# Hidden rows of the expert layer turned by VectorE in 32x32 squares instead of by TensorE

## The reference

```python
logits = xn @ en.T / tau                      # 1536 tokens, 8 experts
expert_idx = np.argmax(logits, axis=1)
gate_w = probs[np.arange(N), expert_idx]
for e in range(E):
    mask = expert_idx == e
    h = np.maximum(x[mask] @ w1[e], 0.0)      # w1: 512 x 1024
    out[mask] = gate_w[mask, None] * (h @ w2[e])   # w2: 1024 x 512
```

## Time and profile before

| | |
|---|---|
| median of three runs | 525.04 us (524.76 to 525.34) |
| profiled execution | 524.4 us, of which the span (first to last instruction) is 522.7 us |
| TensorE busy | 510.8 us, 98% of the span |
| VectorE, ScalarE, GpSimd busy | 332.8, 212.7, 92.6 us |
| mean granted TensorE clock | 0.998 of full |
| share of TensorE in the chain that ended last | 95% |

### The profile page before, as it was taken

The page is one execution under the profiler, slowest core; times in us unless marked ns, Lnnn a source line. Parts: engine busy times, 40 slices in busy tenths (PEclk is TensorE's granted clock), DMA queues, the critical chain, the costliest instruction groups (busy, mean ns, idle before and its releaser), DMA issues.

```text
span 522.7 us, 11557 instructions
## 1 busy us (share of the span) xinstructions
PE 510.8 (98%) x3754; PEld 440.2 (84%) x3755; DVE 332.8 (64%) x712; ACT 212.7 (41%) x480; POOL 92.6 (18%) x223
## 2 busy tenths in 40 slices
PE   8899999999999999999999999999999999999994
PEld 7688888888888888888898988887788888888883
DVE  3779897788876665666654578677573473222662
ACT  5677753443443334333422545440532441111440
POOL 6413131003240000000000001003221211111221
PEclk9999999999999999999999999999999999999999
DMA  8999425587454336332423610102864145101000
GB/s 213 279 334 285 89 56 101 131 152 135 107 129 86 67 66 146 66 66 43 120 42 133 231 41 22 61 3 93 334 250 144 40 184 192 40 29 37 20 20 25
DMA packets 125899, 60.24 MB, mean 115 GB/s; under 512 B 95382, under 2 KB 113814, under 8 KB 125856
## 3 DMA queue, kind: packets, MB, share of 16 engines
q1 hardware_dynamic: 123456, 53.38, 37.8%
q0 software_dynamic: 2400, 6.30, 3.6%
HBM read 50.22 MB, written 11.01 MB: 117 GB/s over the span
## 4 chain that ended last, share of the span: by engine, by line
PE 95%; ACT 1%; issue 1%; DMA 1%; SPq 0%; DVE 0%; POOLq 0%; DVEq 0%; ACTq 0%
PE bank L1050 26%; PE bank L1094 9%; PE bank L1101 9%; PE bank L1107 9%; PE bank L1257 5%; PE bank L1303 5%; PE bank L1265 5%; PE bank L1311 5%; PE bank L1305 5%; PE bank L1259 5%; PE bank L1028 3%; PE bank L998 2%; PE bank L1295 2%; PE bank L1162 1%; PE bank L1007 1%
## 5 line engine op out<-in xcount | busy, mean ns | idle before, releaser
L1458 ACT ACTIVATE el<-bank 128x512 f32<-128x512 f32 x48 | 28.6, 596 | 90.5 <-PE bank L1050 90.2
L1050 PE MATMUL bank<-x_hi,w_hi_parts 128*128 128x256 f32 x376 | 60.5, 283 | 0.0
L1050 PE MATMUL bank<-x_hi,w_lo_parts 128*128 128x256 f32 x376 | 60.2, 282 | 0.0
L1050 PE MATMUL bank<-x_lo,w_hi_parts 128*128 128x256 f32 x376 | 60.1, 282 | 0.0
L1782 DVE TENSOR_SCALAR el<-el 128x512 f32<-128x512 f32 x48 | 20.4, 425 | 59.9 <-ACT el L1458 59.9
L1050 PEld LDWEIGHTS bank<-x_hi,w_hi_parts 128*128 128x128 f32 x376 | 54.1, 188 | 4.1 <-issue 0.2
L1094 PE MATMUL bank<-w_hi_parts,g_hi 128*128 128x512 f32 x192 | 54.5, 405 | 0.0
L1101 PE MATMUL bank<-w_lo_parts,g_hi 128*128 128x512 f32 x192 | 52.6, 395 | 0.0
L1107 PE MATMUL bank<-w_hi_parts,g_lo 128*128 128x512 f32 x192 | 52.4, 394 | 0.0
L789 POOL COPY kb<-kT 128x96 f32<-128x96 f32 x96 | 26.5, 317 | 142.1 <-PE bank L998 120.6
L1050 PEld LDWEIGHTS bank<-x_lo,w_hi_parts 128*128 128x128 f32 x376 | 51.4, 189 | 0.0
(11 more groups left out here) (292 smaller groups left out, 892.1 us busy)
## 6 DMA issues: line engine op xcount, KB each, us to landing
raw<-in_moe_w SPq DMA_DIRECT2D x8, 2048.0 KB
w_raw<-in_moe_w_in SPq DMA_DIRECT2D x8, 512.0 KB, 6.1
w_raw<-in_moe_w_out SPq DMA_DIRECT2D x8, 512.0 KB, 6.6
p_rows<-p_all SPq DMA_DIRECT2D x16, 256.0 KB, 2.4
p_squares<-p_rows SPq DMA_DIRECT2D x64, 64.0 KB, 2.3
v_raw<-in_v SPq DMA_DIRECT2D x8, 384.0 KB, 4.1
x_rows<-x SPq DMA_DIRECT2D x6, 512.0 KB, 3.2
x<-x_rows SPq DMA_DIRECT2D x20, 128.0 KB, 2.7
```

The source lines that it names most:

```text
L1050: mm = pe.matmul(o, r32(w[:, at:at + P]), r32(x[i % 2][:, c, :]), start=(part == "hh" and c == 0), stop=(part == "lh" and c == DC - 1))
L1458: act.activation(el[n % 2], bank[:, H_BANK[n % 2], :], ACT.Exp).then_inc(e_act, 1)
```

## The change

In slots 2 to 13 TensorE's `transpose_h` is gone. VectorE turns the 128x1024 hidden rows out of PSUM with one instruction that transposes each 32x32 block in its place (`turn_h`, into `h_sb`). To complete the turn, the blocks have to change groups of 32 partitions: 16 moves of 32 partitions x 256 elements (`h_square`), 9 by VectorE (`BY_DVE`) and 7 by ScalarE (`BY_ACT`), each with the ReLU in it, into `h_turned_rows`. ScalarE makes `hT_hi` and VectorE `hT_lo` from there (`h_high`, `h_low`). Slots 0 and 1 keep TensorE's turn.

The hidden columns come out in another order, so the rows of w2 are loaded in that order, in four transfers of 32 partitions in place of one of 128. `transpose_x(3)` now stands inside `up(2)`, and `up(3)` runs half by half (`up_by_halves`). On VectorE `store_y(1)` now stands ahead of `store_xsT(3)`. The table has another row (`STARTS_DOWN`): w1 of a run is split three slots ahead of its start (two before), w2 still one slot ahead.

```diff
+    BY_DVE, BY_ACT = SQUARES[0:9], SQUARES[9:16]
...
+        def h_square(r, q):
+            return (h_turned_rows[q * SQ:(q + 1) * SQ, r * GROUPS_OF_F:(r + 1) * GROUPS_OF_F],
+                    h_sb[r * SQ:(r + 1) * SQ, q * GROUPS_OF_F:(q + 1) * GROUPS_OF_F])
...
-                sp.dma_start(raw[:, W1SZ:WSZ].rearrange("p (c n) -> p c n", c=FC2),
-                             w2[bass.ds(ex, 1)].rearrange("o (c p) n -> p (o c) n", p=P)).then_inc(ld_w2, 16)
+                for r in range(GROUPS):
+                    sp.dma_start(raw[r * SQ:(r + 1) * SQ, W1SZ:WSZ].rearrange("p (c n) -> p c n", c=FC2),
```

On TensorE:

```diff
+            up(FILL)
+            up_by_halves(FILL + 1)
+            transpose_x(FILL + 2)
+            down(FILL)
             with pe.Fori(FILL + 1, NSLOT) as s:
                 with pe.If(s < used):
-                    transpose_h(s)
                     with pe.If(s + 1 < used):
                         transpose_x(s + 2)
                         up(s + 1)
                     down(s)
```

On ScalarE:

```diff
+            def move_h(s):
+                act.wait_ge(h_turned, s)
+                act.wait_ge(hT_ev, 2 * s + 2)
+                for r, q in BY_ACT:
+                    to, of = h_square(r, q)
+                    ins = act.activation(to, of, ACT.Relu)
+                ins.then_inc(moved_a, 1)
...
             with act.Fori(FILL, NSLOT) as s:
                 with act.If(s < used):
-                    hT_high(s)
+                    move_h(s)
+                    h_high(s)
+                    there, run = starting_run(act, s + 1, STARTS_DOWN)
                     with act.If(there > 0):
                         high_w2(run())
+                    there, run = starting_run(act, s + 3)
                     with act.If(there > 0):
+                        act.wait_ge(h1_mm, s + 2)
                         high_w1(run())
-                    with act.If(s + 1 < used):
-                        relu(s + 1)
```

On VectorE:

```diff
+            def turn_h(s):
+                dve.wait_ge(h1_mm, s + 1)
+                dve.wait_ge(moved_a, s - FILL)
+                dve.transpose(h_sb, bank[:, 0:2, :].rearrange("p a n -> p (a n)")).then_inc(h_turned, 1)
...
+            with dve.Fori(FILL, NSLOT) as s:
                 with dve.If(s < used):
+                    h_low(s)
+                    with dve.If(s + 1 < used):
+                        turn_h(s + 1)
+                        move_h(s + 1)
+                        store_xsT(s + 2)
+                    there, run = starting_run(dve, s + 1, STARTS_DOWN)
+                    with dve.If(there > 0):
+                        low_w2(run())
+                    there, run = starting_run(dve, s + 3)
+                    with dve.If(there > 0):
+                        low_w1(run())
                     load_gate(s)
                     dve.wait_ge(g_cp, s + 1)
                     store_y(s, gate_cur[:, 0:1])
```

More of the change, by code:

```diff
@@ L160, in build @@
     SQ = 32
+    GROUPS_OF_F = F2 // GROUPS
+    SQUARES = [(r, q) for r in range(GROUPS) for q in range(GROUPS)]
+    BY_DVE, BY_ACT = SQUARES[0:9], SQUARES[9:16]
     O_TURNS = sorted([(q_at(u), 0, u) for u in STEADY if PAIRS < u < BY_SQUARES]
@@ L325, in build @@
          _, _, emb, emb_n,
-         h_sb, hT_hi, hT_lo, slot_vals, _, xs_even) = zone(
+         h_sb, hT_hi, hT_lo, slot_vals, _, xs_even, _, h_turned_rows) = zone(
             "x",
@@ L1279, in up @@
                 pe.wait_ge(xs_hi_v, s + 1)
-                pe.wait_ge(h1_ev, s + 1)
+                if isinstance(s, int) and s == FILL:
+                    pe.wait_ge(h1_ev, FILL + 1)
+                else:
+                    pe.wait_ge(h_turned, s - 1)
                 for c in range(DC):
@@ L1289, in up, with up_by_halves @@
                     up_low(range(HALVES), base).then_inc(h1_mm, 1)
+            def up_by_halves(s):
+                run, base = run_of(pe, s)
+                pe.wait_ge(xs_hi_v, s + 1)
+                pe.wait_ge(xs_ev, s + 2)
+                pe.wait_ge(h_half_turned, 1)
+                for a in range(HALVES):
+                    if a == 1:
+                        pe.wait_ge(h_turned, FILL)
+                    for c in range(DC):
+                        if a == 0:
+                            pe.wait_ge(raw_lo1, QUARTERS * run + (c + 1))
+                        up_high(c, (a,), base, s)
+                    mm = up_low((a,), base, s)
+                mm.then_inc(h1_mm, 1)
             def transpose_h(s):
@@ L1588, in relu, with relu_half @@
                 act.wait_ge(h1_mm, s + 1)
[L1589 to L1592, removed]
+                act.wait_ge(h1_t, 2 * s)
+                relu_half(0)
+                relu_half(1).then_inc(h1_ev, 1)
+            def relu_half(a):
+                rows = h_sb.rearrange("p (c q f) -> p q c f", c=FC2, q=GROUPS)[:, 2 * a:2 * a + 2, :, :]
+                return act.activation(rows, bank[:, a, :].rearrange("p (q c f) -> p q c f", q=2, c=FC2), ACT.Relu)
             def hT_high(s):
@@ L1599, in hT_high, with h_high @@
                              ).then_inc(hT_hi_a, 1)
+            def move_h(s):
[5 more added lines that the diff above has]
+                ins.then_inc(moved_a, 1)
+            def h_high(s):
+                act.wait_ge(moved_a, s - 1)
+                act.wait_ge(moved_d, s - 1)
+                act.wait_ge(h2_mm, s + 1)
+                for a in range(2):
+                    act.copy(r32(of_half(hT_hi, a)), h_by_chunk(a)).then_inc(hT_hi_a, 1)
             def high_w1(run):
@@ L1921, in store_xsT @@
                 dve.wait_ge(xs_t, s + 1)
-                if not isinstance(s, int) or s > 0:
+                if not isinstance(s, int) or s in (1, FILL):
                     dve.wait_ge(h1_mm, s)
-                hi, lo = (x.rearrange("p c n -> p (c n)") for x in (xsT_hi, xsT_lo))
+                hi, lo = (x.rearrange("p c n -> p (c n)") for x in homes_of_turned_rows(s))
                 dve.tensor_copy(r32(hi), bank[:, bank_of_rows(s), :]).then_inc(xs_hi_v, 1)
@@ L2149, in _ @@
                 low_w2(1)
-            store_xsT(3)
             store_y(1, list_gate[:, 0, 1:2])
+            dve.wait_ge(meta_v, 2)
+            store_xsT(FILL + 1)
+            dve.wait_ge(h1_half, 2)
+            dve.wait_ge(h1_t, 2 * FILL)
+            half = F2 // HALVES
+            dve.transpose(h_sb[:, 0:half], bank[:, H1[0], :]).then_inc(h_half_turned, 1)
+            dve.wait_ge(h1_mm, FILL + 1)
+            dve.transpose(h_sb[:, half:F2], bank[:, H1[1], :]).then_inc(h_turned, 1)
+            dve.wait_ge(h_half_turned, 1)
+            dve.wait_ge(r_mm, NB)
+            move_h(FILL)
             there, run = starting_run(dve, slice(3, 4))
@@ L2154, in _ @@
                 low_w1(run())
[L2155 to L2163 removed]
+            there, run = starting_run(dve, slice(4, 5))
+            with dve.If(there > 0):
+                low_w1(run())
             def load_gate(s):
```

123 lines of the change are left out of this document (67 added, 56 removed).

## The result

The changed kernel takes 542.5 us (median of four runs), the kernel before 525.19 on the same chip: ratio 1.0326, 95% interval 1.0304 to 1.0348. It is slower, as forecast, but by 3.3% where 1.8% was forecast, and outside the range (525 to 541) by 1.5 us.

The account below looks back on a forecast made before the run. TensorE, 98% busy, was taken to bound the kernel. Transposes removed -8.7, loop stalls +11.0, tail +5.5, start +0.6, clock +0.9: +9.3 us on the median 525.04, so 534 us (531 to 539 at 0.55), range 525 to 541.

Parts of the forecast that it names:

- turn of 128x1024: VectorE's `turn_h` in each slot: 1.21 us, with 2.05 as bound.
- nine squares: VectorE's moves of 32x256 behind the turn: 0.30 us each without overlap, 2.65 us for nine.
- VectorE's idle before a w2 split: VectorE between the end of `store_xsT` and the low parts of w2: 1.08 us for table reads.
- gap before `down(13)`: TensorE waits 7.1 us between `down(12)` and `down(13)` for `store_y(12)`, where it was 1.62.
- start (`store_y(1)`): At the start, `store_y(1)` waits for the first scatter ahead of `store_xsT(3)`, so `up(3)` starts later: +0.6 us.
- stalls in the loop: TensorE's waits in iterations 2 to 11, mostly from weight splits delaying `store_y` and the next turn: +11.0 us.
- TensorE's own part of the slot: In loop slots, `transpose_x` through `up` stays at 6.01 us; nothing added.
- clock: After the idling in the tail TensorE comes back slower: +0.9 us, half of 1.8; all of `down(13)` slow would be +5.6.
- rival of 0.20: VectorE's squares overlap, 0.20 us each, chain 0.75 shorter in every slot: +3.3 us in all, 528; chance 0.22.
- the part on the plain slot: Slot without a weight split: VectorE's chain takes 5.5 us, TensorE wants `transpose_x` after 5.58: 0.1 us lost a slot.
- TensorE's busy time down by about 9 us: Sign expected in the profile after, with no matmuls on `h_sb` left in the loop.
- The tail: Iteration 12 splits w2 of weight run 3 with no `up` following to hide it: +5.5 us.

Follow-up runs that it names:

- halves: Changed kernel with each of VectorE's nine squares cut into two of 32x128; one execution for its trace, 547.97 us.
- read_first: Changed kernel with TensorE's table read of `up(s+1)` put ahead of `transpose_x(s+2)`; 538.68 us, ratio 1.0270 to the kernel before.
- xs_first: Changed kernel with VectorE's `store_xsT(s+2)` put ahead of its nine squares; 530.67 us, ratio 1.0119 to the kernel before.
- four: Changed kernel with 4 squares on VectorE and 12 on ScalarE in place of 9 and 7; 529.13 us, ratio 1.0100 to the kernel before.
- tail: Changed kernel with the w2 split of weight run 3 moved from iteration 12 to 11; 536.91 us, ratio 1.0243 to the kernel before.
- b5: b1 with the w2 split of weight run 3 moved from iteration 12 to 11; 518.16 us, ratio 0.9881 to the kernel before.
- b1: Changed kernel with xs_first, read_first and four together, and `store_y(1)` back behind `store_xsT(3)` and the half turns; 521.61 us, ratio 0.9951 to the kernel before.
- y_first: Changed kernel with VectorE's `load_gate` and `store_y` of slot s put ahead of the weight splits; 538.95 us, ratio 1.0278 to the kernel before.
- b2: b1 with the low parts of w2 right behind `h_low(s)`, ahead of the turn; 527.54 us, ratio 1.0078 to the kernel before.
- b3: b1 with the gate and `store_y` ahead of the splits on VectorE; 523.54 us, ratio 0.9982 to the kernel before.

## Why the prediction was wrong

**The direction and most of the mechanism were right**: no gain in TensorE's waiting to be had, a chain on VectorE from the end of `up(s+1)` to `store_y(s)`, stalls in the slots with splits, a tail gap. Its pieces:

| step | predicted | measured |
|---|---|---|
| turn of 128x1024 | 1.21 | 1.25 |
| nine squares | 2.65 | 2.66 |
| VectorE's idle before a w2 split | 1.08 | 1.20 |
| gap before `down(13)` | 7.1 | 7.4 |
| ScalarE's seven squares | 2.6 | 2.97 |
| start (`store_y(1)`) | +0.6 | +0.65 |
| stalls in the loop | +11.0 | +7.9 |
| TensorE's own part of the slot | 0 | +7.7 |
| clock | +0.9 | +3.7 |

**The rule on squares held.** The Trainium skill ("VectorE: DVE Perf Modes", section "Two Vector instructions with no wait between them") says that an instruction in another group of 32 partitions is held until all earlier ones have finished. The squares start 0.296 us apart and last 0.283, and `halves` shows 0.22 with and 0.145 without a change of partitions. The prediction's 0.30 a square stands, and its rival of 0.20 falls. Its reason is not quite right: it says that each square reads and writes other partitions than the last, but up to four in a row read the same ones, and only where they write changes. The trace agrees with the rule as cited, by which either is enough.

**The step that failed** is in the part on the plain slot: "TensorE wants its `transpose_x` 5.58 after the end of `up`, and needs some 0.2 to react: 0.1 us lost a slot." It took the rest of TensorE's slot, 6.01 from `transpose_x` through `up`, as fixed, and priced a late `xsT_lo` at the wait for it alone. But the sequencer's read of `tab` stands behind that wait. With `transpose_x` released only when TensorE gets to it the read can't start sooner, and each slot pays 0.81 more, 7.7 us in the loop. read_first shows that this is the read, xs_first and four that it is paid only while `xsT_lo` comes late: they have no transposes of `h_sb` either and pay nothing. The eight transposes would have given the read 0.87 us more time; the prediction removed them at their full cost and counted no such loss. By the same step its sign "TensorE's busy time down by about 9 us" failed: it fell by 1.

**The stalls of the loop** were over-estimated as a consequence. TensorE was 0.8 us later in each slot, so `y_sb` was less late for it. With the read moved away (read_first) the stalls are 12.6 us against the 11.0 forecast, so the stepping through the slots was near for the TensorE that it assumed. One error thus partly hid the other: together they are 15.6 where 11.0 stood.

**The clock** is the second term that was mis-sized: +0.9 predicted for the tail, +2.2 measured there. Nothing was put down for `up(3)`, where a wait of 2.0 us was followed by another 1.5 lost. The prediction's 3.6 us at half clock were the better figure than the half of it that was taken: in `down(13)` the granted clock is 0.50 for over 4 us. It read them from the distance of matmuls at the start of the program alone; the table of stretches gives a granted clock of 1.00 there (0 to 4 us). By the Trainium skill ("TensorE: Matmul & The Clock Gate", section "HAM oscillation — how this bites in real kernels"), as the prediction told it, the whole 1.8 would have been lost in the tail; the trace shows that and a little more. Not every wait of some us did so: 3.1 us before `up(3)` in `tail` and 2.1 before `down(13)` in b5 cost nothing.

**The tail** was right in mechanism and in size (5.5 and 5.8), and `tail` and b5 show how much of it is the place of one split: the wait falls from 7.25 to 3.27 us, and from 4.64 to 2.10.

What stays open: the +1.1 us up to `up(2)`, which come and go between variants with the same code, and why a wait of two or three microseconds lowers the clock in one place and not in another (below).

## What to carry to other kernels

Before removing work from the bound engine, list what its sequencer does between the instructions, reads of registers from memory first: a read behind an instruction whose wait ends only as the engine gets there is paid (here 0.81 us a slot), so read ahead of the wait, or let what it waits for come earlier. When work goes to a second engine in program order, put there first what the bound engine wants soonest (here the next slot's rows, 2.7 us earlier for a swap of two lines), and move big jobs without a deadline, such as splits of weights, to an iteration that has something to hide them. Such edits win together: none of the single ones beat the kernel before, while b1 and b5 do. Reordering alone can also only move a wait: y_first, b2 and b3 took from one place what they gave in another.

## What the runs showed of the hardware

- A read of a table in SBUF by an engine's sequencer cost TensorE 0.81 us a slot where nothing covered it. On VectorE two in a row cost 1.2 to 1.4 us and three 2.1 (changed), behind the squares 0.4 to 0.7 and 1.35 (xs_first), and two 0.2 to 0.6 in b1.
- A square of 32x256, SBUF to SBUF, takes 0.415 us on ScalarE and 0.283 on VectorE; the turn of 128x1024 out of PSUM takes 1.25 us on VectorE.
- The clock after a wait, by how long `down(13)` then took (5.8 us at full clock) and by `up(3)` to `transpose_x(4)` (5.6):

| wait before it, us | kernel, phase | time of the phase, us |
|---|---|---|
| 0.7 | b1, `up(3)` | 5.6 |
| 2.0 | changed, `up(3)` | 7.2 |
| 2.4 | xs_first, `up(3)` | 7.1 |
| 2.4 | halves, `up(3)` | 5.6 |
| 3.1 | tail, `up(3)` | 5.6 |
| 2.1 | b5, `down(13)` | 5.8 |
| 3.3 | tail, `down(13)` | 7.4 |
| 4.6 | b1, `down(13)` | 8.3 |
| 7.25 | changed, `down(13)` | 8.1 |

The length of the wait alone doesn't decide: before `up(3)`, 3.1 us left the clock up in one kernel and 2.0 lowered it in another, and 2.4 us did either. Nor does the drop come at once. After the 3.3 us of `tail` the first matmuls of `down(13)` (from 521.49) ran at full clock and the next at half (the granted clock is the 0.80 and the 0.50):

```profile
521.00:524.00 3.00, 2.52 (x9) 2.01 (x10) 1.41 (x4) 0.00 (x0) 1.19 (x1) 0.80 0.06 22
524.00:526.00 2.00, 2.00 (x6) 1.61 (x5) 0.00 (x0) 0.00 (x0) 0.19 (x1) 0.50 0.06 24
```
